# Reordering the start of a delta-rule attention and two mixture-of-experts layers on one Trainium2 core

## The chip, the cores and the metric

The kernel runs on one core of one Trainium2 chip. The metric is the device time of one launch in microseconds (us). TensorE is called PE here, its weight load PEld, VectorE DVE, ScalarE ACT, GpSimd POOL and SyncE SP. SPq and ACTq are the issue slots of SP and ACT, in which those engines start DMA transfers.

## The reference, cut to what matters

Three layers follow one another. The first is a linear attention with a delta rule, over 4 batches x 8 heads, 768 positions, head size 48. The second sends its output through 8 experts, all of them for all tokens, weighted by a matrix that is balanced 8 times over rows and columns. The third sends every token through its best expert only.

```python
def _attn_ref(q, k, v, beta):
    k_n = k / (np.linalg.norm(k, axis=-1, keepdims=True) + 1e-06)
    for t in range(S):
        y[:, :, t] = einsum('bhd,bhde->bhe', q[:, :, t], state)
        v_old = einsum('bhde,bhd->bhe', state, kt)
        state = state + bt * einsum('bhd,bhe->bhde', kt, vt - v_old)

def _moe_ref(x, w_gate, w1, w2):            # N, D, E, F = 3072, 384, 8, 1024
    P = np.exp(logits - logits.max())
    for _ in range(8):
        P /= P.sum(1); P /= P.sum(0); P *= N / E
    for e in range(E):
        out += P[:, e:e + 1] * (np.maximum(x @ w1[e], 0.0) @ w2[e])

def _moe2_ref(x, expert_emb, tau, w1, w2):
    # cosine score against 8 embeddings, argmax, softmax weight of the winner
    out[mask] = gate_w[mask, None] * (np.maximum(x[mask] @ w1[e], 0.0) @ w2[e])
```

## The kernel before, in words

The attention is cut into NC = 12 chunks of C = 64 positions; the 32 heads lie as 16 pairs, two heads on the 128 partitions. For a chunk `c` the kernel makes:

- `gram(c)`, the 64x64 products of keys with keys (64 small matmuls into `psA`), which `scale(c, ...)` on DVE multiplies by `gam` and stores as `an`; SP writes it to memory in `store_a(c)`.
- `mix(c)`, the products of keys with queries (64 small matmuls into `psH` or `psB`). ACT copies the result to `mt[c]` in `copy_m(c)`, DVE masks it in `mask(c)`.
- The inverse of a triangular matrix. Two chunks together are a group `n`. SP loads their 32x32 blocks in `load_blocks(n)` (tile `sa`, 8 loads of 64 KB), DVE solves in `solve(n, first, end)` (31 steps of two instructions, lines 945 and 948), ACT transposes in `transpose_blocks(n)` (tile `sr`), SP stores in `store_inverse(n)`, and `load_inverse(engine, c)` loads the blocks back in another layout (tiles `rs`, `ts`, 6 loads of 64 KB a chunk).
- `cross(c)` and `corner(c)`, which make the off-diagonal block of the inverse, then `write_values(c)`, `outputs(c)`, `keys_state(c)`, which carry the state from chunk to chunk, and `transpose_y(c)`, `scores(c)` with `high_x` on ACT and `low_x` on DVE, which hand the chunk's output to the second layer.

`gam` holds the inverse squared norms of the keys times beta. The keys come in PARTS = 6 parts of 768 KB (`load_parts(m)`, tiles `kq`); ACT squares them (`squares_of(m)`), DVE sums them (`reduce_part(m)`), ACT takes the root (`root(i)`), DVE finishes (`norms(i)`). Parts 3 to 5 are finished together, in `norms(3)`.

The first expert of the second layer is computed chunk by chunk beside the attention: `block_hidden(k)` (nine matmuls, line 1392) and `block_give(k)` (six matmuls, line 1407), 8 of each for a chunk. Each weight is used as a high and a low part: `split_first(half, layer)` on ACT makes the high part from the loaded `fh` (line 641), the one on DVE the low part (line 980). The other seven experts and the third layer follow.

The order is written out by hand. Before the main loop each engine runs a prologue; then every engine walks `for s in range(LAST)` and does at step `s` what the tables `AT_KS`, `AT_X`, `AT_O`, `AT_W`, `AT_Y`, `AT_T`, `AT_SC`, `AT_GRAM`, `AT_MIX`, `AT_MASK`, `AT_PART`, `AT_SPLIT` and `SOLVE` place there. Each engine is in order, and engines meet only through semaphores. Chunk 0 has `cross` at s=0, `corner` at 1, `write_values` at 2, `outputs` at 3; chunk 1 has `cross` at 2, `corner` at 3, `keys_state` at 4, `outputs` at 6; `block_hidden(0)` is at s=6. `gram(4)`, `gram(5)` and `gram(6)` are at 8, 9 and 14. `mix(4)` to `mix(7)` are at 1, 2, 4 and 5. Within one step of PE the block products come first, then `keys_state`, `transpose_y`, `scores`, `cross`, `corner`, `write_values`, `outputs`, `gram`, `mix`.

Keys and queries for `gram` and `mix` of the first eight chunks come in pairs of chunks, 1 MB each, into the buffers `kP[0..2]` and `qP[0..1]`: pair 2 of the queries reuses `qP[0]`, pair 3 reuses `kP[1]` and `qP[1]`. From `gram(6)` on, keys come chunk by chunk into `kTs`.

SP issues nearly all transfers in one order. In the main loop it has at s=9 `store_inverse(1)`, at s=10 `store_a(4)`, then these lines, then `load_inverse` for chunks 2 and 3, at s=11 `store_a(5)`, and at s=12 `load_blocks(2)` and the load of `kTs` that `gram(6)` waits for:

```python
if s == AT_GRAM[5] + 1:
    sp.wait_ge(g_done, 6)
    sp.wait_ge(m_done, 8)
    sp.wait_ge(y_done, 2)
    for m in range(3, PARTS):
        load_parts(m)
```

Of the kernel before, what the change touches and what calls it, by code (L numbers as in the profile page):

```python
# [15 lines left out]
P = 128  # L16
C = 64
NC = S // C
# [4 lines left out]
KC = DM // P  # L23
# [44 lines left out]
AT_SOLVED = [None, 8] + [16 * n - 9 for n in range(2, NG)]  # L68
AT_MASK = [None, 2] + [t + 1 for t in AT_KS[2:]]

EARLY = 4
AT_MIX = [None] * EARLY + [1, 2, 4, 5] + [AT_KS[c - 4] + 4 for c in range(8, NC)]
AT_GRAM = [None] * EARLY + [8, 9, AT_KS[2] + 3] + [AT_KS[c - 4] + 2 for c in range(7, NC)]
AT_PART = [None] * 3 + [11, 12, 13]
AT_SPLIT = {2: (0, 0), 3: (0, 1), 5: (1, 0), 6: (1, 1)}
AT_SPLIT_END = 7
# [36 lines left out]
def build(nc, kT, qT, kn, vn, beta, consts, wg, w1, w2, emb, tau, v1, v2, out):  # L113
# [5 lines left out]
    with ExitStack() as ctx:  # L119
# [6 lines left out]
        def keep(name, shape, dt=F32, at=None):  # L126
            if at is None:
                at = top[0]
                top[0] += -(-4 * int(np.prod(shape[1:])) // 32) * 32
            return nc.alloc_sbuf_tensor_at(name, shape, dt, offset=at)  # L130
# [4 lines left out]
        for i in range(2):  # L135
# [13 lines left out]

        part, pair = 4 * 2 * NJ * D, 4 * GR * NJ * C  # L150
        kq = [keep(f"kq{i}", [P, 2 * NJ, D], at=at) for i, at in
              enumerate([w_at, w_at + part, w_at + 3 * part] + [x_at + (2 + i) * part for i in range(3)])]
        assert part == 4 * 2 * KC * SLOT
# [8 lines left out]
        kP = [keep(f"kP{i}", [P, GR, NJ, C], at=x_at + i * pair) for i in range(KP)]  # L162
        qP = [keep(f"qP{i}", [P, GR, NJ, C], at=x_at + NC * (chunk_x - chunk_m) + 8 * chunk_m + i * pair) for i in range(2)]

# [154 lines left out]
        def mix_bank(c):  # L319

            return psA if c >= 8 else psB if c in (1, 3) else psH
# [45 lines left out]
        with nc.Block() as block:  # L367
            @block.sync
            def _(sp):
# [7 lines left out]
                def store_a(c):  # L377
                    sp.wait_ge(an_ready, c + 1)
                    sp.dma_start(a_dram[c], an[a_buffer(c)][:, :, :]).then_inc(an_out[a_buffer(c)], 16)
# [49 lines left out]
                load_pair(qP[1], qT, 1, s_qP[1])  # L429
                load_first(0)  # L430
                for c in range(2):
                    load_corner(c)
                store_a(2)
                sp.dma_start(kns[:, :, :], kn[0]).then_inc(s_kn, 16)
                sp.dma_start(kTs[:, :, :], kT[1]).then_inc(s_kT, 16)
                sp.dma_start(qTs[:, :, :], qT[1]).then_inc(s_qT, 16)
                load_parts(2)
                sp.dma_start(embs[0:E, :], emb).then_inc(emb_in, 16)
                sp.dma_start(wgs[:, :, :], wg.rearrange("(k p) e -> p k e", p=P)).then_inc(s_wg, 16)
                sp.dma_start(taus[:, :], tau.to_broadcast([P, 1])).then_inc(tau_in, 16)  # L440
                load_pair(kP[2], kT, 2, s_kP[2])
                sp.wait_ge(m_done, 2)
                load_pair(qP[0], qT, 2, s_qP[0])
                store_inverse(0)
                store_a(3)
                load_blocks(1)
                load_first(1)
                sp.wait_ge(vs_ready, 1)
# [3 lines left out]
                load_pair(kP[1], kT, 3, s_kP[1])  # L452
                load_pair(qP[1], qT, 3, s_qP[1])
                for s in range(LAST):
                    if s - 2 in AT_GRAM[EARLY:6]:
                        store_a(AT_GRAM.index(s - 2))
                    if s - 2 in AT_GRAM[6:NC]:
                        store_a(AT_GRAM.index(s - 2))
                    if s == AT_GRAM[5] + 1:
                        sp.wait_ge(g_done, 6)  # L460
                        sp.wait_ge(m_done, 8)
                        sp.wait_ge(y_done, 2)
                        for m in range(3, PARTS):
                            load_parts(m)
                    if s == 12:
# [139 lines left out]
            def _(act):  # L605
# [17 lines left out]
                def copy_m(c):  # L623
                    act.wait_ge(m_done, c + 1)
                    act.activation(mt[c][:, :, :], mix_bank(c)[:, :, :], ACT.Copy).then_inc(mt_copied, 1)

# [22 lines left out]
                root(1)  # L649
                for c in range(1, EARLY):  # L650
                    copy_m(c)
                squares_of(2)
                transpose_blocks(0)
                for c in range(2):
                    load_inverse(act, c)

# [205 lines left out]
            def _(dve):  # L862
# [169 lines left out]
                solve(0, 0, BS - 1)  # L1032
                scale(3, psA)

                first_iteration = AT_SC[-1] + 2
                for s in range(LAST):
# [8 lines left out]
                    if k is not None:  # L1045
                        low(k)
                    if s == AT_SPLIT_END - 2:
                        reduce_part(2)
                    if s == AT_SPLIT_END + 1:
# [222 lines left out]
            def _(pe):  # L1272
# [149 lines left out]
                pe.wait_ge(mt_copied, 2)  # L1422
                mix(3)
                pe.wait_ge(s_const, 16)
                pe.wait_ge(s_wg, 16)
                for s in range(LAST):
# [28 lines left out]
                    if s in AT_MIX:  # L1455
                        c = AT_MIX.index(s)
                        if c >= 8:
                            pe.wait_ge(an_ready, c + 1)
                        else:
                            pe.wait_ge(mt_copied, c - 1 if c == 4 else c)  # L1460
                        mix(c)
# [192 lines left out]
```

## Time and profile before

| what | value |
| --- | --- |
| time, median of 3 runs | 2381.35 us (2379.86 to 2382.3) |
| the profiled execution's own time | 2386.1 us |
| its span, first to last instruction | 2384.2 us |
| PE busy in the span | 2253.3 us (95%) |
| DVE, ACT, POOL busy in the span | 1020.9, 612.3, 106.2 us |
| mean granted clock of PE, share of full speed | 0.959 |

A start is counted from the span's start. "Idle before" is the time in which the engine did nothing ahead of an instruction, with what ended it. The granted clock of PE has two levels, 2.4 GHz (1.00 in a row) and 1.2 GHz (0.50); a value between them is a mean over a stretch. Times of a page belong to one execution, the median to unprofiled ones.

### The profile page before, as it was taken

The numbers are of one execution on the slowest core, as the hardware profiler recorded it, in microseconds if no ns is written. First come the engines' busy times: TensorE is split into PE (matmuls) and PEld (weight loads), VectorE is DVE, ScalarE is ACT, GpSimd is POOL, SyncE is SP. The second block draws the span as 40 slices with busy tenths as digits, with TensorE's granted clock in tenths as the row PEclk, the third lists the DMA queues.
The fourth block names the chain that finished last, engine by engine and source line by source line (L and its number), as shares of the span: only waits on it lengthen the run. The fifth ranks groups of instructions, "written<-read, shape, count | busy, mean of one in ns | idle before, by whom it ended". The sixth has DMA issues, their size and how long they took to land.

```text
span 2384.2 us, 43062 instructions
## 1 busy us (share of the span) xinstructions
PE 2253.3 (95%) x18100; PEld 2090.3 (88%) x18100; DVE 1020.9 (43%) x1831; ACT 612.3 (26%) x1021; POOL 106.2 (4%) x106
## 2 busy tenths in 40 slices
PE   3779999999999999999999999999999996899998
PEld 3768898998999998999899899989999886899998
DVE  6655555435333332333333232332323225566664
ACT  2322222322111111111111111111111112566664
POOL 0000000000000000000000000000000000222221
PEclk7779999999999999999999999999999997899999
DMA  8544434331000000000000000000000012666651
GB/s 283 128 140 130 128 115 116 110 143 53 1 27 1 27 10 18 27 1 27 1 27 27 1 27 1 27 27 1 1 1 1 23 31 96 218 217 219 232 194 61
DMA packets 153379, 173.93 MB, mean 73 GB/s; under 512 B 82124, under 2 KB 113008, under 8 KB 153218
## 3 DMA queue, kind: packets, MB, share of 16 engines
q1 hardware_dynamic: 142018, 158.50, 20.7%
q0 software_dynamic: 4864, 12.20, 1.4%
q8 instruction: 137, 2.24, 0.4%
q10 hardware_dynamic: 6336, 0.79, 0.3%
q14 instruction: 24, 0.20, 0.0%
HBM read 145.50 MB, written 28.71 MB: 73 GB/s over the span
## 4 chain that ended last, share of the span: by engine, by line
PE 89%; DVE 5%; DMA 2%; SPq 1%; issue 1%; ACT 0%; ACTq 0%; POOL 0%; POOLq 0%; DVEq 0%
PE psA L1491 21%; PE psH L1506 15%; PE psB L1491 8%; PE psB L1506 7%; PE psY L1506 7%; PE psY L1600 7%; PE psH L1392 4%; PE psA L1276 4%; PE psA L1587 3%; PE psY L1407 3%; PE psB L1587 3%; PE psB L1365 1%; PE psB L1375 1%; DVE products L945 1%; DVE sx L948 1%
## 5 line engine op out<-in xcount | busy, mean ns | idle before, releaser
L1491 PE MATMUL psA<-X,wh 128*128 128x512 f32 x1440 | 456.3, 398 | 6.2 <-DVE wl L1092 4.1
L1099 DVE SCALAR_TENSOR_TENSOR hl<-psA,hh 128x512 fp32r<-128x512 f32 x240 | 166.1, 692 | 649.5 <-ACT hh L769 649.4
L769 ACT ACTIVATE hh<-psA 128x512 fp32r<-128x512 f32 x240 | 143.8, 599 | 856.6 <-PE psA L1491 856.6
L1491 PEld LDWEIGHTS psA<-X,wh 128*128 128x128 f32 x1440 | 270.6, 191 | 53.3 <-issue 7.7
L1491 PE MATMUL psA<-X,wl 128*128 128x512 f32 x720 | 289.2, 402 | 0.0
L1506 PE MATMUL psH<-wh,hh 128*128 128x384 f32 x672 | 228.4, 340 | 0.0
L1506 PE MATMUL psH<-wh,hl 128*128 128x384 f32 x672 | 227.2, 338 | 0.0
L1506 PE MATMUL psH<-wl,hh 128*128 128x384 f32 x672 | 225.8, 336 | 0.0
L1099 DVE SCALAR_TENSOR_TENSOR hl<-psB,hh 128x512 fp32r<-128x512 f32 x96 | 66.5, 693 | 277.2 <-ACT hh L769 277.2
L1491 PE MATMUL psB<-X,wh 128*128 128x512 f32 x576 | 179.2, 392 | 0.0
L1223 DVE TENSOR_TENSOR vl<-vs,vh 128x768 fp32r<-128x768 f32 x152 | 145.1, 957 | 57.4 <-ACT vh L806 55.8
L1491 PEld LDWEIGHTS psA<-X,wl 128*128 128x128 f32 x720 | 137.5, 191 | 29.8
L769 ACT ACTIVATE hh<-psB 128x512 fp32r<-128x512 f32 x96 | 57.5, 599 | 344.0 <-PE psB L1491 344.0
L806 ACT ACTIVATE vh<-vs 128x768 fp32r<-128x768 f32 x152 | 127.3, 840 | 15.0 <-DMA vs<-v_d 14.9
L1506 PEld LDWEIGHTS psH<-wh,hh 128*128 128x128 f32 x672 | 126.3, 188 | 0.0
L1506 PEld LDWEIGHTS psH<-wl,hh 128*128 128x128 f32 x672 | 126.1, 188 | 0.0
L1506 PEld LDWEIGHTS psH<-wh,hl 128*128 128x128 f32 x672 | 125.9, 187 | 0.0
L1491 PEld LDWEIGHTS psB<-X,wh 128*128 128x128 f32 x576 | 106.7, 188 | 17.7
L1392 PE MATMUL psH<-X,wh 128*128 128x256 f32 x576 | 116.3, 298 | 1.2 <-DVE X L975 1.2
L1491 PE MATMUL psB<-X,wl 128*128 128x512 f32 x288 | 114.0, 396 | 0.0
L1506 PE MATMUL psB<-wh,hl 128*128 128x384 f32 x336 | 113.9, 339 | 0.0
L1506 PE MATMUL psB<-wl,hh 128*128 128x384 f32 x336 | 113.7, 338 | 0.0
(235 smaller groups left out, 4247.8 us busy)
## 6 DMA issues: line engine op xcount, KB each, us to landing
vs<-v_d SPq DMA_DIRECT2D x38, 768.0 KB, 6.2
vs<-v_d SPq DMA_DIRECT2D x19, 1536.0 KB, 12.2
ws<-w_d SPq DMA_DIRECT2D x28, 768.0 KB, 6.2
kT<-kT_d SPq DMA_DIRECT2D x17, 512.0 KB, 4.3
qT<-qT_d SPq DMA_DIRECT2D x15, 512.0 KB, 5.1
a_scratch<-an SPq DMA_DIRECT2D x12, 512.0 KB, 3.5
kq<-kn_d SPq DMA_DIRECT2D x6, 768.0 KB, 8.1
vn<-vn_d SPq DMA_DIRECT2D x12, 384.0 KB, 4.4
```

The source lines that it names most:

```text
L769: act.activation(hh[kk % 3][:, :], ps_h[kk % (2 if last else 3)], ACT.Relu).then_inc(hh_ready, 1)
L806: act.activation(piece(to, q), piece(src, q), ACT.Copy).then_inc(vh_ready, 1)
L945: dve.tensor_tensor(pv, sa[n % 2][:, s + 1:BS, s:s + 1].to_broadcast([P, rows, cols]), sx[:, s:s + 1, 0:cols].to_broadcast([P, rows, cols] ...
L1099: dve.scalar_tensor_tensor(hl[b][:, :], ps_h[bank], 0.0, hh[b][:, :].bitcast(F32), ALU.max, ALU.subtract).then_inc(hl_ready, 1)
L1223: dve.tensor_tensor(piece(to, q), piece(src, q), piece(high, q).bitcast(F32), ALU.subtract).then_inc(vl_ready, 1)
L1276: mm = pe.matmul(ps[g * C:g * C + M, j, at:at + W], lhsT[g * C:g * C + K, j, 0:M], rhs[g * C:g * C + K, j, 0:W], start=True, stop=True, sk ...
L1392: mm = pe.matmul(ps_b[k % 2], a[half][:, c, col], X[:, u, b, c, :], start=(n == 0), stop=(n == 3 * KC - 1))
L1407: mm = pe.matmul(ps_u[i], a[k % 4][:, i * P:(i + 1) * P], b[half][:, f % FB, :], start=(f == 0 and n == 0), stop=(f == KF - 1 and n == 2))
L1491: mm = pe.matmul(to, a[half][:, c, col], X[:, 2 * g:2 * g + 2, b, c, :], start=(n == 0), stop=(n == 3 * KC - 1))
L1506: mm = pe.matmul(ps_y[i][:, 0:DM], a[kk % 3][:, q], b[half][:, f, :], start=(f == 0 and n == 0), stop=(f == FB - 1 and n == 2))
L1587: mm = pe.matmul(ps_g[f % 4], a[par][:, c, f * P:(f + 1) * P], b[par][:, c, :], start=(n == 0), stop=(n == 3 * KC - 1))
L1600: mm = pe.matmul(ps_o[s], a[f % 4][:, q], b[par][:, f, :], start=(f == 0 and n == 0), stop=(f == KF - 1 and n == 2))
```

## The change

In PE's prologue `mix(4)` and `mix(5)` are added behind `mix(3)`, ahead of `cross(0)`; `mix(6)` and `mix(7)` take their places at s=1 and 2. For that SP loads pair 2 right behind query pair 1, and ACT copies all six results in its prologue. ACT and DVE split the first half of the first expert's weights in their prologues, and DVE masks chunk 1 and reduces part 2 there; the second half is split at s=8 and 9. SP now issues the six inverse loads of chunk 1 that ACT issued, ahead of `load_blocks(1)`; the loads of `qTs` for chunk 1 and of the second half of the weights (`load_first(1)`) move behind pair 3. Parts 3 to 5 of the keys are loaded at s=7 instead of 10, into other addresses, and worked on at s=9 to 11 instead of 11 to 13, so that `norms(3)` is at s=13 instead of 15. `copy_m(8)` has a wait for all six reductions.

```diff
--- before.py
+++ after.py
@@ -66,13 +66,13 @@
 SOLVE_SECOND = [4, 4, 4, 4, 3, 3, 3, 3, 3]
 SOLVE_THIRD = [2, 3, 3, 3, 3, 3, 3, 3, 3, 3, 2]
 AT_SOLVED = [None, 8] + [16 * n - 9 for n in range(2, NG)]
-AT_MASK = [None, 2] + [t + 1 for t in AT_KS[2:]]
+AT_MASK = [None, None] + [t + 1 for t in AT_KS[2:]]
 
 EARLY = 4
-AT_MIX = [None] * EARLY + [1, 2, 4, 5] + [AT_KS[c - 4] + 4 for c in range(8, NC)]
+AT_MIX = [None] * 6 + [1, 2] + [AT_KS[c - 4] + 4 for c in range(8, NC)]
 AT_GRAM = [None] * EARLY + [8, 9, AT_KS[2] + 3] + [AT_KS[c - 4] + 2 for c in range(7, NC)]
-AT_PART = [None] * 3 + [11, 12, 13]
-AT_SPLIT = {2: (0, 0), 3: (0, 1), 5: (1, 0), 6: (1, 1)}
+AT_PART = [None] * 3 + [9, 10, 11]
+AT_SPLIT = {8: (1, 0), 9: (1, 1)}
 AT_SPLIT_END = 7
 AT_EMB = 18
 SPILLED = 10
@@ -148,8 +148,9 @@
         end_dense = top[0]
 
         part, pair = 4 * 2 * NJ * D, 4 * GR * NJ * C
+        late_at = x_at + NC * (4 * 2 * KC * SLOT - 4 * NJ * C) + 8 * 4 * NJ * C
         kq = [keep(f"kq{i}", [P, 2 * NJ, D], at=at) for i, at in
-              enumerate([w_at, w_at + part, w_at + 3 * part] + [x_at + (2 + i) * part for i in range(3)])]
+              enumerate([w_at, w_at + part, w_at + 3 * part, late_at, late_at + part, x_at + 4 * part])]
         assert part == 4 * 2 * KC * SLOT
         fh1 = [keep(f"fh1_{i}", [P, KC, FH], at=wl_at + 4 * KC * FH * i) for i in range(2)]
         fh2 = [keep(f"fh2_{i}", [P, FB, DM], at=wl_at + 8 * KC * FH + 4 * FB * DM * i) for i in range(2)]
@@ -160,7 +161,7 @@
         chunk_x, chunk_m = 4 * 2 * KC * SLOT, 4 * NJ * C
         mt = [keep(f"mt{c}", [P, NJ, C], at=x_at + NC * (chunk_x - chunk_m) + c * chunk_m) for c in range(NC)]
         kP = [keep(f"kP{i}", [P, GR, NJ, C], at=x_at + i * pair) for i in range(KP)]
-        qP = [keep(f"qP{i}", [P, GR, NJ, C], at=x_at + NC * (chunk_x - chunk_m) + 8 * chunk_m + i * pair) for i in range(2)]
+        qP = [keep(f"qP{i}", [P, GR, NJ, C], at=late_at + i * pair) for i in range(2)]
 
         top[0] = base
         kTs, qTs = keep("kT", [P, NJ, C]), keep("qT", [P, NJ, C])
@@ -427,41 +428,42 @@
                 load_blocks(0)
                 sp.dma_start(vns[:, :, :], vn[0]).then_inc(s_vn, 16)
                 load_pair(qP[1], qT, 1, s_qP[1])
-                load_first(0)
+                load_pair(kP[2], kT, 2, s_kP[2])
+                sp.wait_ge(m_done, 2)
+                load_pair(qP[0], qT, 2, s_qP[0])
                 for c in range(2):
                     load_corner(c)
                 store_a(2)
+                load_first(0)
+                load_parts(2)
                 sp.dma_start(kns[:, :, :], kn[0]).then_inc(s_kn, 16)
                 sp.dma_start(kTs[:, :, :], kT[1]).then_inc(s_kT, 16)
-                sp.dma_start(qTs[:, :, :], qT[1]).then_inc(s_qT, 16)
-                load_parts(2)
                 sp.dma_start(embs[0:E, :], emb).then_inc(emb_in, 16)
                 sp.dma_start(wgs[:, :, :], wg.rearrange("(k p) e -> p k e", p=P)).then_inc(s_wg, 16)
                 sp.dma_start(taus[:, :], tau.to_broadcast([P, 1])).then_inc(tau_in, 16)
-                load_pair(kP[2], kT, 2, s_kP[2])
-                sp.wait_ge(m_done, 2)
-                load_pair(qP[0], qT, 2, s_qP[0])
                 store_inverse(0)
                 store_a(3)
+                load_inverse(sp, 1)
                 load_blocks(1)
-                load_first(1)
                 sp.wait_ge(vs_ready, 1)
                 sp.dma_start(vns[:, :, :], vn[1]).then_inc(s_vn, 16)
                 sp.wait_ge(m_done, 4)
                 sp.wait_ge(g_done, 4)
                 load_pair(kP[1], kT, 3, s_kP[1])
                 load_pair(qP[1], qT, 3, s_qP[1])
+                sp.dma_start(qTs[:, :, :], qT[1]).then_inc(s_qT, 16)
+                load_first(1)
                 for s in range(LAST):
                     if s - 2 in AT_GRAM[EARLY:6]:
                         store_a(AT_GRAM.index(s - 2))
                     if s - 2 in AT_GRAM[6:NC]:
                         store_a(AT_GRAM.index(s - 2))
-                    if s == AT_GRAM[5] + 1:
-                        sp.wait_ge(g_done, 6)
+                    if s == 7:
                         sp.wait_ge(m_done, 8)
+                        load_parts(3)
+                        load_parts(4)
                         sp.wait_ge(y_done, 2)
-                        for m in range(3, PARTS):
-                            load_parts(m)
+                        load_parts(5)
                     if s == 12:
                         load_blocks(2)
                     if s in range(24, 16 * NG - 24, 16):
@@ -622,6 +624,8 @@
 
                 def copy_m(c):
                     act.wait_ge(m_done, c + 1)
+                    if c == 8:
+                        act.wait_ge(s_red, PARTS)
                     act.activation(mt[c][:, :, :], mix_bank(c)[:, :, :], ACT.Copy).then_inc(mt_copied, 1)
 
                 def transpose_blocks(n):
@@ -647,12 +651,13 @@
                 squares_of(1)
                 copy_m(0)
                 root(1)
-                for c in range(1, EARLY):
+                for c in range(1, 6):
                     copy_m(c)
+                split_first(0, 0)
+                split_first(0, 1)
                 squares_of(2)
                 transpose_blocks(0)
-                for c in range(2):
-                    load_inverse(act, c)
+                load_inverse(act, 0)
 
                 def high_x(c):
                     act.wait_ge(t_done, c + 1)
@@ -1031,6 +1036,10 @@
                 mask(0)
                 solve(0, 0, BS - 1)
                 scale(3, psA)
+                mask(1)
+                split_first(0, 0)
+                split_first(0, 1)
+                reduce_part(2)
 
                 first_iteration = AT_SC[-1] + 2
                 for s in range(LAST):
@@ -1044,8 +1053,6 @@
                     k = block_of(s)
                     if k is not None:
                         low(k)
-                    if s == AT_SPLIT_END - 2:
-                        reduce_part(2)
                     if s == AT_SPLIT_END + 1:
                         norms(2)
                     if s - 1 in AT_PART:
@@ -1421,6 +1428,10 @@
                 mix(2)
                 pe.wait_ge(mt_copied, 2)
                 mix(3)
+                pe.wait_ge(mt_copied, 3)
+                mix(4)
+                pe.wait_ge(mt_copied, 5)
+                mix(5)
                 pe.wait_ge(s_const, 16)
                 pe.wait_ge(s_wg, 16)
                 for s in range(LAST):
@@ -1457,7 +1468,7 @@
                         if c >= 8:
                             pe.wait_ge(an_ready, c + 1)
                         else:
-                            pe.wait_ge(mt_copied, c - 1 if c == 4 else c)
+                            pe.wait_ge(mt_copied, c)
                         mix(c)
                     if s == AT_SC[-1]:
                         pe.wait_ge(rt, RT_EN)
```

## Rows read from the trace of the kernel before

**Rows 1.** Busy time of each engine by stretch; last columns: PE clock, DMA share, GB/s

```profile
36.60:65.10 28.50, 0.01 (x1) 0.04 (x3) 15.23 (x40) 4.46 (x3) 0.00 (x0) 0.55 1.00 249
...
68.00:72.00 4.00, 0.47 (x18) 0.48 (x20) 3.79 (x9) 1.18 (x2) 0.89 (x1) 0.50 1.08 375
...
125.00:154.50 29.50, 20.47 (x331) 19.34 (x332) 11.89 (x18) 9.19 (x13) 0.00 (x0) 0.79 0.78 220
600.00:2384.00 1784.00, 1741.06 (x9464) 1605.97 (x9463) 695.36 (x1098) 448.08 (x761) 80.49 (x78) 0.98 0.16 52
```

**Rows 2.** Timeline of PE, 60 to 170 us: start, duration, instruction, idle before

```profile
65.09 1.92 PE L1334 MATMUL psB<-rs,ao 32*32 32x32 f32 x64 [28.50 <-issue]
...
79.28 1.92 PE L1334 MATMUL psB<-rs,ao 32*32 32x32 f32 x64 [2.23 <-DMA rs<-r_scratch]
...
106.43 0.48 PE L1392 MATMUL psH<-X,wh 128*128 128x256 f32 x2 [1.17 <-DVE X L975]
...
118.25 2.08 PE L1276 MATMUL psA<-kP 48*64 48x64 f32 x64
...
125.05 3.68 PE L1276 MATMUL psA<-kP 48*64 48x64 f32 x64 [2.42 <-DVE an L927]
...
154.52 3.68 PE L1276 MATMUL psA<-kT 48*64 48x64 f32 x64 [7.28 <-DMA kT<-kT_d]
...
168.39 0.66 PE L1407 MATMUL psY<-wh,hhA 128*128 128x384 f32 x1 [4.96 <-DVE y0s L967]
```

**Rows 3.** Timeline of DVE, 60 to 166 us

```profile
65.33 0.21 DVE L945 TENSOR_TENSOR products<-sa,sx 128x31 f32<-128x31 f32 x1 [8.34 <-issue]
...
101.66 1.75 DVE L980 TENSOR_TENSOR wl<-fh,wh 128x1536 fp32r<-128x1536 f32 x1
103.33 2.23 DVE L975 TENSOR_TENSOR X<-xf,X 128x768 fp32r<-128x768 f32 x1
105.48 1.74 DVE L889 TENSOR_REDUCE n<-kq 128x32 f32<-128x1536 f32 x1
...
118.65 0.95 DVE L975 TENSOR_TENSOR X<-xf,X 128x768 fp32r<-128x768 f32 x1
...
161.21 0.20 DVE L898 TENSOR_SCALAR n<-n 128x96 f32<-128x96 f32 x1
...
164.43 1.22 DVE L927 TENSOR_TENSOR an<-psA,gam 128x1024 f32<-128x1024 f32 x1
```

**Rows 4.** Timeline of SP's DMA issues, 60 to 230 us: start, time of issuing

```profile
63.09 0.47 SPq L375 DMA_DIRECT2D qP<-qT_d  x1
...
125.55 0.33 SPq L403 DMA_DIRECT2D r_scratch<-sr  x1
...
128.77 2.16 SPq L372 DMA_DIRECT2D kq<-kn_d  x3
...
142.88 1.03 SPq L361 DMA_DIRECT2D rs<-r_scratch  x2
...
150.15 0.48 SPq L474 DMA_DIRECT2D kT<-kT_d  x1
...
220.57 0.32 SPq L361 DMA_DIRECT2D rs<-r_scratch  x1
...
227.68 1.02 SPq L361 DMA_DIRECT2D rs<-r_scratch  x2
```

**Rows 5.** Timeline of ACT with its DMA issues, 50 to 71 us

```profile
50.97 1.95 ACT L634 ACTIVATE sr<-sx 128x1024 f32<-128x1024 f32 x1 [5.46 <-DVE sx L948]
...
63.17 7.05 ACTq L361 DMA_DIRECT2D rs<-r_scratch  x2
```

**Rows 6.** The query pairs' tile, 0 to 160 us: time from issue to landing

```profile
DMA to landing us min/median/max: 6.9/9.8/14.9
```

**Rows 7.** The chain that ended last, 52 to 56 us

```profile
52.95 2.68 DMA r_scratch<-sr
```

**Rows 8.** Timeline of POOL, 0 to 210 us

```profile
102.70 2.05 POOL L561 TENSOR_TENSOR vn<-vn,br 128x768 f32<-128x768 f32 x1 [29.83 <-DMA vn<-vn_d]
```

## The prediction

> **What bounds the kernel now.** I read the stretches first. From 600 us on PE is busy in 1741.1 of 1784 us [rows 1], and the change touches nothing there; that part can only shift as a block. Then I looked on PE's timeline for idle time in the first 170 us, where all moved work lies. PE has nothing to do from 36.6 to 65.1 us, while DVE solves the first group (15.2 us busy) and ACT is busy for 4.5 us [rows 1]. The other gaps are a wait for the inverse of chunk 1 at 79.28 us (2.23 us), for DVE's `low_x` at 106.43 (1.17), for DVE's `scale(4)` at 125.05 (2.42), for the keys of `gram(6)` at 154.52 (7.28) and for DVE's `unit_out(0)` at 168.39 (4.96) [rows 2]. So the start is bound by a chain that changes engine at every step, and what counts is which wait ends last at each of these places. Behind 168 us PE, the engine that ends last, keeps its order and its work, so I carry the shift at 168.39 to the end of the span unchanged.
>
> **Part 1, the products ahead of `cross(0)`, and pair 3.** `mix(4)` and `mix(5)` fall into the idle 28.5 us of PE: 3.68 us each at the slower clock (a `gram` has the same 64 matmuls and lasts that long in [rows 2]), so they cost nothing. ACT gets two copies, two splits and nothing else new before its transpose at 50.97 us. It is free 5.46 us ahead of that now [rows 5] and idle for most of the 30 us before (4.5 us busy of 28.5 [rows 1]), which covers it if the weights land in time; with the cover gone each us late would be a us on everything behind. DVE's moved mask (the size of the 1.22 us at 164.43), two splits and one reduction (1.2 + 2 x 1.75 + 1.74 = 6.5 us) fit ahead of 65.33 us, up to which it is idle for 8.34 us behind its memsets [rows 3].
>
> At s=1 PE now meets `mix(6)`, which stands in front of `cross(1)` and needs pair 3. This is the new wait, and I look for what ends it. Before, the query pair 3 was issued at 63.09 us [rows 4] and landed 14.9 us later (the longest of the four [rows 6]), at 78.0. Ahead of it in SP's queue stood 1.5 MB of weights, `load_first(1)`, now behind it. At 375 GB/s [rows 1] they take 4.2 us. The small loads ahead of the pair are 20 in either order (12 of inverses, 8 of blocks). So pair 3 lands at 73.8, `mix(6)` runs to 77.5, and `cross(1)` starts 1.8 us earlier than at 79.28; its own inverse loads, now ahead of the pair in the queue, are there by then. The bounds: not before `corner(0)` is done, about 70 us (65.09 and 1.92 for `cross(0)` [rows 2], ACT's copy, as much again for `corner(0)`; ACT no longer issues loads until 70.22 [rows 5]), and not behind the 78.0 of before if only the order changes. I take 73.8, since both ends need the same bytes to move. Behind the waiting `mix(6)` stand all of PE's work, and through it everything. The blocks of group 1 land some 4 us later than for 65.33 us, as six more loads are ahead of them; DVE's first 16 steps then end before 85, when PE has delivered nothing to it yet. The cost is nothing.
>
> **Part 2, s=4 to s=9.** PE loses two products of 2.08 us here [rows 2]. DVE loses more: the split at 101.66 (1.75 us), the reduction at 105.48 (1.74) and both splits of the second half (2 x 1.75), which now stand behind `scale(4)` and `scale(5)` [rows 3]. Without the split, `low_x(0)` starts at 101.66 instead of 103.33. There it took 2.23 us, the next one 0.95 [rows 3], and POOL worked from 102.70 on [rows 8]; if it starts at 101.66 it is done before POOL begins. So `block_hidden(0)` starts at 102.7 instead of 106.43, 3.7 us earlier; if the stall of 1.28 us stays on it, 2.4. I take 3.7, the sum so far being 5.5. The first split stood where DVE waited for PE, and its removal is counted at nothing.
>
> The Trainium skill, in "SBUF — State Buffer", section "SBUF: two separate sides", calls the port pair of VectorE and GpSimd an exclusive lock held for the whole instruction. The 2.23 against 0.95 us agree with it; whoever starts first wins, which is the order assumed here, and with POOL first the sum would be 1.3 us less.
>
> From `block_hidden(0)` to the end of `gram(4)` (106.43 to 120.33) PE ran without a wait and does so again, 5.5 us earlier. `scale(4)` was then late by DVE's backlog: PE waited 2.42 us. With 5.2 us less on DVE it waits only for what hangs on the last block: its copy, `low(3)` and `scale(4)`, the last alone 1.22 us (as at 164.43 [rows 3]), less what PE does beside it. What stays of the 2.42 lies between nothing and all; I take 1.0, near the 1.22. So `gram(5)` starts at 118.1, 6.9 us earlier. The two splits now run on DVE beside `gram(5)` and the blocks behind it, and the first is needed at `block_hidden(4)`, 2.1 to 3.7 us after `scale(4)` has ended, against 1.75 for its run. That costs nothing; uncovered it would cost up to 1.75.
>
> **Part 3, SP's queue up to `gram(6)`.** `gram(6)` waits for a load issued at 150.15 [rows 4]. SP came to it late. The end of the solve and the transposed blocks come about 7.0 us earlier by part 2 (125.55 becomes 118.5). Their store lands 2.68 us after its issue [rows 7], at 128.2 before, but SP then issued the three parts of the keys until 130.93 and only then the twelve inverse loads: 2.7 us go away. These twelve took from 130.93 to 143.91, 13.0 us, with 2.3 MB of keys in front of them; the next time, without, 8.1 us (220.57 to 228.70) [rows 4]. I take 8.1, saving 4.9; the other bound is 0, if the issue is slow by itself. Then `store_a(5)`, `load_blocks(2)` and the keys follow unchanged. Sum: 7.0 + 2.7 + 4.9 = 14.6 us, `gram(6)` at 139.9. Is PE there? Its work from 125.05 to 154.5 is 20.5 us [rows 1]; from 118.1 that ends at 138.6. So the load still ends last, by a little over a us, and a slip of PE beyond that would be the next bound. The parts' own loads now go out at s=7, where SP has little else to issue; one of them stands ahead of `kns` and `qTs` of chunk 2, which nobody reads before `outputs(2)` at s=18. The added wait of `copy_m(8)` is at s=31, long after the reductions.
>
> On DVE the reductions of parts 3 to 5 now stand at s=10 to 12. The first (1.74 us) is ahead of `scale(5)`, which SP's `store_a(5)` needs only when its twelve loads are out, so it is hidden.
>
> **Part 4, `unit_out(0)`.** Between `gram(6)` and 168.39 lay `norms(3)`, from 161.21 to 164.43 [rows 3], 3.2 us in the middle of the chain to `unit_out(0)`, for which PE waited 4.96 us. At s=13 it now runs while PE waits for the keys. The gain is 3.2, bounded by 0 if the reduction or root comes late. Sum: 14.6 + 3.2 = 17.8 us. The profiled span would go from 2384.2 to 2366.4 us, its own time from 2386.1 to 2368.3. The median was 4.75 below that own time, so I subtract from the median: 2381.35 - 17.8 = 2363.55, say 2363.6 us.
>
> **The rivals.**
> A: the twelve loads are slow by themselves. For it: the last two of ACT's twelve took 7.05 us [rows 5]; against: the 8.1 us of the second set. It takes back 4.9: 2368.5 us.
> B: pair 3 lands where it did, at 78.0, because the small loads and not the bytes set it. It takes back 4.2, and everything behind it shifts: 2367.8 us.
> C: PE's clock stays up. `gram(6)` took 3.68 us behind an idle 7.28, the same product 2.08 at 118.25 behind busy work [rows 2]. The wait shrinks to about 1.3 us. At full clock `gram(6)` gains 1.6 us, and the block products behind it and at 168 us some 2.4 more (an estimate, by the same ratio from about 5.5 us of slow work): 4.0 in all, 2359.6. Against it, `gram(5)` was slow behind only 2.42 us of idle.
> D, the other side: `mix(6)` is a new gate. Every us that pair 3 is late beyond 73.8 is a us lost; at 91.6 the gain is gone, from 96.4 on the kernel is slower by over 0.2%. SP has 14 small loads ahead of the pair, from 55.63 on, when the first inverse has landed [rows 7]. At the pace of ACT's last two, 3.5 us each [rows 5], they end at 104.7, and with 6.7 us for the 2.5 MB behind them `mix(6)` starts at 111.4: 19.8 us slower, 2401.2. At 0.5 us each, as the last two of [rows 4], they end near 63.
> E: nothing is won: the earlier start is given back to waits at s=19 and later: 2381.4.
>
> On C the Trainium skill ("TensorE: Matmul & The Clock Gate", section "What's actually happening") says that the slow clock is the default and activity releases it. By that, shorter waits help beyond their length, and C would be the outcome at 2359.6; the trace agrees in that long gaps are followed by slow products.
>
> **How the numbers follow.** Forecast 0.56, A 0.12, B 0.10, C 0.12, D 0.04, E 0.06. All but D and E are faster by over 0.2% (4.8 us, about what a measurement of this kernel can tell from no change): faster 0.90, same 0.06, slower 0.04. The low end is C with an early pair 3 (2 us more), 2357.5; the high end is A and B together, 2372.7. It leaves out D and E.
>
> **What would show it.** In the new trace: `mix(4)` and `mix(5)` before 50 us; `mix(6)` starting near 74 behind a wait for the query or key pair; no wait for inverse loads at `cross(1)`; `block_hidden(0)` near 101; `gram(5)` near 118; twelve loads in about 8 us; `gram(6)` near 140 still behind a wait for keys; the first product into `psY` of chunk 1 near 150.6 with under 2 us of idle. It would be wrong if the transpose at 50.97 moved, if `mix(6)` started behind 78, or if a gap opened behind 170 us that is not there now.

## The result and the profile after

The changed kernel took 2364.76 us (median of 4 runs, 2361.99 to 2368.86) against 2381.82 us before: ratio 0.9931, 95% interval 0.9914 to 0.9948, 17.1 us less. Run again unaltered it gave 2363.22 us against 2381.26, ratio 0.9927 (0.9914 to 0.9941), 18.0 us less. The forecast was 2363.6 us, 17.8 less.

The timeline of PE after, 0 to 175 us, has these rows where [rows 2] had theirs; `mix(4)` and `mix(5)` come first, `cross(0)` third, `mix(6)` fourth, and the last is `cross(3)`, which stood at 197.17 us before:

```profile
36.29 2.10 PE L1283 MATMUL psH<-qP,kP 48*64 48x64 f32 x64
39.51 2.08 PE L1283 MATMUL psH<-qP,kP 48*64 48x64 f32 x64 [1.12 <-ACT mt L629]
60.53 1.92 PE L1341 MATMUL psB<-rs,ao 32*32 32x32 f32 x64 [18.95 <-issue]
...
71.64 3.68 PE L1283 MATMUL psH<-qP,kP 48*64 48x64 f32 x64 [5.98 <-DMA qP<-qT_d]
75.24 1.92 PE L1341 MATMUL psB<-rs,ao 32*32 32x32 f32 x64
...
95.27 1.50 PE L1327 MATMUL psB<-wgs,xf 128*128 128x8 f32 x12 [0.90 <-ACT xf L671]
...
99.38 0.79 PE L1399 MATMUL psH<-X,wh 128*128 128x256 f32 x2
...
117.56 2.08 PE L1283 MATMUL psA<-kP 48*64 48x64 f32 x64 [1.12 <-DVE an L932]
...
137.63 2.76 PE L1283 MATMUL psA<-kT 48*64 48x64 f32 x64 [1.71 <-DMA kT<-kT_d]
...
147.23 0.41 PE L1414 MATMUL psY<-wh,hhA 128*128 128x384 f32 x1 [2.64 <-DVE y0s L972]
...
174.20 1.92 PE L1341 MATMUL psB<-rs,ao 32*32 32x32 f32 x64 [3.23 <-DVE pm L1071]
```

Each gap of [rows 2] is shorter or gone. New are 5.98 us for pair 3 ahead of `mix(6)`, 0.90 us ahead of `scores(0)`, 0.80 us ahead of `keys_state(2)` at 124.86, and the 1.12 us ahead of `mix(5)`, which costs nothing, as PE waits 18.95 us behind it. The last row waits for the same 3.23 us as in the kernel before, so from there the order runs as it did.

SP's issues after, 117 to 134 us, against [rows 4]: the blocks are stored 7.8 us earlier, no keys stand behind them, and the twelve inverse loads run from 120.91 to 127.07, in 6.2 us:

```profile
117.73 0.33 SPq L404 DMA_DIRECT2D r_scratch<-sr  x1
...
120.91 0.32 SPq L362 DMA_DIRECT2D rs<-r_scratch  x1
...
126.05 1.02 SPq L362 DMA_DIRECT2D rs<-r_scratch  x2
...
133.37 0.48 SPq L476 DMA_DIRECT2D kT<-kT_d  x1
```

DVE after around `low_x(0)` (line 980 of the changed kernel), against [rows 3]; and POOL's product of the same time, against [rows 8]:

```profile
98.09 0.95 DVE L980 TENSOR_TENSOR X<-xf,X 128x768 fp32r<-128x768 f32 x1
...
99.92 1.56 DVE L950 TENSOR_TENSOR products<-sa,sx 128x231 f32<-128x231 f32 x1
```

```profile
99.54 1.68 POOL L563 TENSOR_TENSOR vn<-vn,br 128x768 f32<-128x768 f32 x1 [33.09 <-DMA vn<-vn_d]
```

`low_x(0)` ran before POOL began and took 0.95 us; the stall went to a product of the solve (1.56 us, its neighbours 0.40). The Trainium skill ("SBUF — State Buffer", section "SBUF: two separate sides") says that whichever of the two engines starts first gets the shared port pair for its whole instruction. The trace agrees: the product that began 0.38 us behind POOL's start took 1.16 us longer than its neighbours.

### The profile page after: what moved, and what is told of

The parts are those of the page before. It is cut to its first block, busy times and chain, and to the rows that moved or that the text cites. A ratio compares the mean times of both kernels' runs of the same rounds, so it can differ in the third digit from the quotient of the medians.

```text
span 2360.2 us, 43063 instructions
## 1 busy us (share of the span) xinstructions
PE 2249.2 (95%) x18100; PEld 2086.9 (88%) x18100; DVE 1021.7 (43%) x1831; ACT 611.9 (26%) x1021; POOL 105.2 (4%) x106
## 4 chain that ended last, share of the span: by engine, by line
PE 90%; DVE 5%; DMA 2%; SPq 1%; issue 1%; ACT 1%; POOL 0%; POOLq 0%; DVEq 0%; ACTq 0%
PE psA L1502 21%; PE psH L1517 15%; PE psB L1502 8%; PE psB L1517 7%; PE psY L1517 7%; PE psY L1611 7%; PE psH L1399 4%; PE psA L1598 4%; PE psB L1598 3%; PE psY L1414 3%; PE psA L1283 3%; PE psB L1372 1%; PE psB L1382 1%; SPq L398 1%; DVE products L950 1%
## 5 line engine op out<-in xcount | busy, mean ns | idle before, releaser
L811 ACT ACTIVATE vh<-vs 128x768 fp32r<-128x768 f32 x152 | 127.1, 839 | 15.1 <-DMA vs<-v_d 15.0
## 6 DMA issues: line engine op xcount, KB each, us to landing
vs<-v_d SPq DMA_DIRECT2D x19, 1536.0 KB, 12.1
```

The source lines that it names most:

```text
L811: act.activation(piece(to, q), piece(src, q), ACT.Copy).then_inc(vh_ready, 1)
```

## How far two executions differ

The first profiled execution of the kernel before took 2386.1 us, 5 us above its median, and that of the changed kernel 2361.99, 3 us below. A shift read from the two alone comes out at 24 us. So both kernels were run and profiled once more.

> The kernel before, unaltered, once more, for a second profile. Its first profiled execution took 2386.1 us, its median is 2381. If the 5 us lie in the start, cross(3) starts at 190 to 193 us here instead of 197.2, and its span ends near 2379.

> The changed kernel once more, unaltered, for a second profile and a tighter ratio. If the 23 us by which cross(3) (line 1341 after the third chunk) was earlier in the first profile (174.2 against 197.2 us) belongs to the change, it starts at 173 to 176 us again and the ratio is near 0.990. If 5 to 6 us of it were the luck of two single executions, as the medians (17 us apart) say, it starts at 176 to 180 us in this profile, or the later part of the span is longer, and the ratio is 0.9925 to 0.9935.

The second execution of the kernel before took 2379.18 us, with a span of 2377.3; `cross(3)` started at 193.92 us instead of 197.17, so 3 of the 7 us between the two lie in the first 197 us; the start lies 0.9 us above the expected range. The second of the changed kernel had a span of 2359.9 and `cross(3)` at 175.80, as expected if all of the shift belonged to the change, while its ratio, 0.9927, is that of the other case. Both profiled executions of the changed kernel (2361.99 and 2361.72 us) were faster than their medians. Start times in us, as means of two executions each:

| place | before | after | earlier by | forecast |
| --- | --- | --- | --- | --- |
| `cross(1)` | 79.28, 77.73 | 75.24, 76.43 | 2.7 | 1.8 |
| `block_hidden(0)` | 106.43, 103.99 | 99.38, 100.56 | 5.2 | 5.5 |
| `gram(5)` | 125.05, 122.96 | 117.56, 117.93 | 6.3 | 6.9 |
| `gram(6)` | 154.52, 151.49 | 137.63, 138.19 | 15.1 | 14.6 |
| first product of `block_give(8)` | 168.39, 165.36 | 147.23, 148.83 | 18.8 | 17.8 |
| `cross(3)` | 197.17, 193.92 | 174.20, 175.80 | 20.5 | 17.8 |
| end of the span | 2384.2, 2377.3 | 2360.2, 2359.9 | 20.7 | 17.8 |

Single executions differ by 1 to 4 us at these places, so a row confirms a term only to about that. The timed runs say 17.1 and 18.0 for the whole.

## Experiments

All were timed against the kernel before on the same chip; all but the second profile of the kernel before have an interval. These intervals reach some 3 us to either side, so a difference between two changed kernels, taken from their ratios, is known to 4 or 5 us only. Where it is no larger, the start times in the profiles have to carry the reading.

**Parts of the keys alone.** In the kernel before:

```diff
-AT_PART = [None] * 3 + [11, 12, 13]
+AT_PART = [None] * 3 + [9, 10, 11]
-                    if s == AT_GRAM[5] + 1:
-                        sp.wait_ge(g_done, 6)
+                    if s == 7:
...
```

with the new addresses and the wait in `copy_m(8)`.

> The kernel before with parts 3 to 5 of the keys alone moved (their new addresses, loads at s=7, squares at s=9 to 11, norms(3) at s=13). Theory (SP's queue): gram(6) loses its late keys, 7.6 us of queue time, but cannot start before PE is ready, 7.3 us earlier than 154.5; norms(3) leaves the chain to unit_out(0), 3.2 us. Sum 10.5, less up to 1.7 for the reduction ahead of scale(5): 2371 to 2373 us. Rival (the queue is not the gate, the gain comes from the products and the splits): at most 3 us, 2379 us.

Measured: 2373.75 us, ratio 0.9970 (0.9958 to 0.9982), 7.1 us faster. `gram(6)` started at 146.59 us behind a wait of 0.92, and `block_give(8)` waited 2.98 us instead of 4.96 or 5.19. The mechanism holds; the time is 0.8 us above the expected range, and the wait at `block_give(8)` shrank by 2.0 to 2.2 us where 3.2 were expected.

**The parts put back** into the changed kernel (the reverse of that diff, the addresses kept).

> The changed kernel with parts 3 to 5 loaded at s=10 and worked on at s=11 to 13 again. Theory (SP's queue): the twelve inverse loads take 13 us again instead of 8, and 2 to 3 us go to issuing the keys; gram(6) starts 7 to 8 us later than in the changed kernel, and norms(3) adds 3.2: 2374 to 2376 us. Rival (other waits end last there, the parts are hidden): within 3 us of the changed kernel.

Measured: 2376.72 us, ratio 0.9977 (0.9968 to 0.9986), 12 us slower than the changed kernel by the ratios, where 10 to 11 were expected; so the rest of the change alone is worth 5.5 us (3.3 to 7.6 by the interval). SP's issues of this kernel, 121 to 146 us:

```profile
121.89 0.33 SPq L404 DMA_DIRECT2D r_scratch<-sr  x1
...
123.84 1.63 SPq L373 DMA_DIRECT2D kq<-kn_d  x3
125.59 0.40 SPq L362 DMA_DIRECT2D rs<-r_scratch  x1
...
126.64 4.17 SPq L362 DMA_DIRECT2D rs<-r_scratch  x1
...
131.52 4.31 SPq L362 DMA_DIRECT2D rs<-r_scratch  x3
...
137.46 1.02 SPq L362 DMA_DIRECT2D rs<-r_scratch  x2
...
143.76 1.79 SPq L476 DMA_DIRECT2D kT<-kT_d  x1
```

Single loads take up to 4.17 us to issue here, and the twelve end at 138.48, 12.9 us after they began; with the parts at s=7 they took 6.2. `gram(6)` waited 5.91 us for its keys and started at 149.13, 27.4 us behind `gram(5)` where it was 20.1 and 20.3; that is the expected 7 to 8 us. This excludes rival A, that the loads are slow by themselves. The two halves alone give 7.1 and 5.5 us, together 17 to 18. With the parts alone PE itself came late to `gram(6)` (146.59, wait 0.92); with the rest alone its keys did (149.13, wait 5.91); only with both does it start at 137.63 and 138.19.

**The late `norms(3)`.**

```diff
-AT_PART = [None] * 3 + [9, 10, 11]
+AT_PART = [None] * 3 + [11, 12, 13]
```

> The changed kernel with the early loads of parts 3 to 5, but squares, reductions and norms(3) at s=11 to 15 as before. Theory: gram(6) stays (137 to 139 us), the 3.2 us of norms(3) come back between gram(6) and unit_out(0), PE's wait for y0s grows by as much: 3.2 us slower than the changed kernel. Rival: the wait for y0s has another cause (the 3 solve steps and the low part), then no difference.

Measured: 2370.41 us, ratio 0.9952 (0.9938 to 0.9965), about 6 us slower than the changed kernel. The wait for `y0s` is 5.87 us instead of 2.64 and 2.20, 3.2 to 3.7 more, as expected. The rest is not explained in full. In this profile `gram(5)` was late already (121.37 us), behind a longer fall of PE's clock, of which below. But `gram(6)`, expected at 137 to 139, came at 143.69 behind a wait of 4.80 us for its keys, 22.3 us behind `gram(5)` instead of 20.1 and 20.3; whether the edit has a part in that is open.

**The weights ahead of pair 3 again.**

```diff
                 load_blocks(1)
+                load_first(1)
...
-                load_first(1)
                 for s in range(LAST):
```

> The changed kernel with the load of the second half of the first expert's weights (1.5 MB) ahead of pair 3 again. Theory (bytes ahead of the pair, each us of mix(6) is a us of the kernel): mix(6) starts 4.2 us later, and so does everything behind, the end too: 4 us slower than the changed kernel. Rival (the small loads set the landing, or the lateness is taken up by a later wait): mix(6) or at least gram(6) where it was, no difference.

Measured: 2370.25 us, ratio 0.9949 (0.9935 to 0.9964), 5.2 us slower than the changed kernel. `mix(6)` started at 78.30 us instead of 71.64 and 72.82, behind a wait of 11.19 us, and `gram(6)` at 144.94 instead of 137.63 and 138.19, 6.8 to 7.3 later. So `mix(6)` is a gate that passes its lateness on, and 1.5 MB ahead of the pair cost 5.5 to 6.7 us there, more than the 4.2 of the forecast.

**Chunk 1's inverse loads on ACT again.**

```diff
-                load_inverse(sp, 1)
...
-                load_inverse(act, 0)
+                for c in range(2):
+                    load_inverse(act, c)
```

> The changed kernel with the six inverse loads of chunk 1 on ACT's queue again. Theory: ACT issues until 60 to 66 us, behind big transfers up to 70, so the copy between cross(0) and corner(0) is late, but mix(6) waits for pair 3 anyway (71.6 us): no difference or, as SP gets to pair 3 some 3 us sooner, 1 to 3 us faster. Rival (the move is what made cross(1) free of its wait): cross(1) waits for inverse loads again, 2 us or more slower.

Measured: 2368.89 us, ratio 0.9949 (0.9937 to 0.9961), 5.2 us slower; the theory of the expectation was wrong, and its rival came out. PE's timeline of this kernel, 60 to 83 us:

```profile
65.31 1.92 PE L1341 MATMUL psB<-rs,ao 32*32 32x32 f32 x64 [23.17 <-issue]
70.98 1.92 PE L1349 MATMUL psB<-xx,ts 32*32 32x32 f32 x64 [3.76 <-ACT xx L728]
72.83 3.68 PE L1283 MATMUL psH<-qP,kP 48*64 48x64 f32 x64
80.97 1.91 PE L1341 MATMUL psB<-rs,ao 32*32 32x32 f32 x64 [4.46 <-DMA rs<-r_scratch]
```

Pair 3 is there when `mix(6)` comes, but `cross(1)` waits 4.46 us for its inverse loads, and starts 4.5 to 5.7 us later than in the changed kernel. The move from ACT to SP is what frees it. On SP's queue these loads stand ahead of the big transfers; on ACT's they run beside them, and I take their late landing to come from that, though only the landing was seen. The same move frees chunk 0: `cross(0)` follows the store of its inverse by 12.3 us here (12.1 and 12.2 in the kernel before) and by 9.2 and 9.1 in the changed kernel, and `corner(0)` waits 3.76 us for ACT's copy here instead of 1.29.

**`mix(6)` and `mix(7)` behind `cross(1)`.**

```diff
-AT_MIX = [None] * 6 + [1, 2] + ...
+AT_MIX = [None] * 6 + [2, 3] + ...
```

> The changed kernel with mix(6) and mix(7) one step later (s=2 and 3), so that cross(1) and write_values(0) no longer stand behind the wait for pair 3. Theory (mix(6) is the new gate): cross(1) starts near 66 to 68 us instead of 75.2, the wait moves behind write_values(0) and shrinks; what comes after is 4 to 5 us earlier, the kernel 4 us faster than the changed one. Rival (the gate is something else, a load of cross(1) or DVE's solve): under 1 us.

Measured: 2359.78 us, ratio 0.9908 (0.9893 to 0.9922), about 4.5 us faster than the changed kernel, where 4 were expected; the intervals of the two just overlap. `cross(1)` started at 68.67 us, a little above the expected 66 to 68, and `mix(6)` at 73.97 without a wait.

**The second splits ahead of `scale(4)` again.**

```diff
-AT_SPLIT = {8: (1, 0), 9: (1, 1)}
+AT_SPLIT = {5: (1, 0), 6: (1, 1)}
```

> The changed kernel with the two splits of the second half of the weights at s=5 and 6 again, ahead of scale(4). Theory (DVE's backlog): 3.5 us more on DVE before scale(4); PE's wait ahead of gram(5) grows from 1.1 us by 2 to 3.5, and all behind it is that much later, the kernel 2 to 3.5 us slower. Rival (the queue of SP alone sets gram(6)): gram(5) late, gram(6) in place, under 1 us.

Measured: 2367.24 us, ratio 0.9939 (0.9924 to 0.9954), 2.8 us slower by the middle of the interval, which overlaps that of the changed kernel. PE waited 2.41 us ahead of `gram(5)` (at 120.75) instead of 1.12; from the start of `gram(4)` to that of `gram(5)` it took 6.80 us instead of 5.51. The mechanism is seen at 1.3 us of the 2 to 3.5; on the end the runs don't settle it. `gram(6)` was not in place but at 142.65, so the rival, that SP's queue alone sets it, did not come out.

**PE's clock where two products are gone.** Here are the busy times by stretch, with the clock granted to PE in the third column from the right: 97 to 103 and 103 to 114 us of the kernel before, of the changed one, and of the one with the parts put back, in this order.

```profile
97.00:103.00 6.00, 6.00 (x146) 5.69 (x143) 5.62 (x9) 2.68 (x3) 0.30 (x1) 1.00 0.46 156
103.00:114.00 11.00, 9.83 (x287) 9.54 (x284) 10.66 (x19) 5.78 (x6) 1.74 (x1) 1.00 0.16 53
```

```profile
97.00:103.00 6.00, 6.00 (x123) 5.78 (x121) 5.76 (x12) 1.20 (x2) 1.68 (x1) 0.72 0.86 322
103.00:114.00 11.00, 11.00 (x254) 10.91 (x248) 8.03 (x25) 4.61 (x7) 0.00 (x0) 1.00 0.45 158
```

```profile
97.00:103.00 6.00, 6.00 (x82) 5.89 (x81) 5.73 (x12) 1.04 (x2) 1.66 (x1) 0.61 0.26 88
103.00:114.00 11.00, 11.00 (x219) 10.72 (x219) 5.41 (x15) 2.59 (x5) 0.00 (x0) 0.75 0.25 85
```

The clock fell to 0.50 (1.2 GHz) for 3.4 us in the changed kernel and for 10.2 in the other, behind the 0.90 us wait and the twelve products of `scores(0)`, where `mix(6)` had stood ahead of `scores(0)` and `mix(7)` behind it. It fell there in all seven profiles with both products at s=1 and 2, in four of them for 3.4 us, in two for 10.2 and in one for 13.7, and in none of the three in which they stand at the old places. From the start of `keys_state(1)` to that of `gram(4)` it took 20.5 us in the changed kernel, 23.5 with the parts put back and 25.1 with the loads on ACT, without any difference in PE's work.

Three more kernels put `mix(7)` at s=4, between `transpose_y(0)` and `scores(0)`, where the wait is; `mix(6)` stands at s=3, 2 and 1 in them, so that the third moves `mix(7)` alone:

```diff
+AT_MIX = [None] * 6 + [3, 4] + ...
+AT_MIX = [None] * 6 + [2, 4] + ...
+AT_MIX = [None] * 6 + [1, 4] + ...
```

> The changed kernel with mix(6) at s=3 and mix(7) at s=4, between transpose_y(0) and scores(0), where PE waits 0.9 us for ACT's copy. Theory: as with mix(6) and mix(7) at s=2 and 3, cross(1) starts near 68.5 us, and one product fills the wait ahead of scores(0): equal to that variant or up to 1 us faster, 2358 to 2360 us. Rival: chunk 1 waits longer for the copies, up to 2 us slower than that variant.

> The changed kernel with mix(6) at s=2, behind write_values(0), and mix(7) at s=4, between transpose_y(0) and scores(0). Theory: 2358 to 2360 us, as above, block_hidden(0) near 93 us. Rival: copy and product at s=4 delay scores(0) and chunk 1's values by more than the wait they fill, 1 to 2 us slower.

> The changed kernel with mix(7) alone moved, from s=2 to s=4. In every profile of the changed kernel PE's granted clock fell to 0.50 near 97 us for 3 to 13 us, where mix(6) and mix(7) stood before, and in none of the kernel before. Theory: sparse work of PE there lets the clock fall; with mix(7) put back there is no fall from 96 to 110 us, or a shorter one, and the runs scatter less (3 us instead of 7). In sum 1 to 3 us faster than the changed kernel, and gram(4) at most 22.5 us behind the start of keys_state(1) (20.5 in the shortest case). Rival: the fall is a chance of the execution; the clock falls here as well and the time is that of the changed kernel or up to 2 us more.

| kernel | median, us | ratio (interval) | `cross(1)` | `block_give(8)` | clock, 97 to 103 us |
| --- | --- | --- | --- | --- | --- |
| changed, again | 2363.22 | 0.9927 (0.9914 to 0.9941) | 76.43 | 148.83 | 0.72 |
| `mix` 6, 7 at s=2, 3 | 2359.78 | 0.9908 (0.9893 to 0.9922) | 68.67 | 141.01 | 1.00 |
| at 3, 4 | 2360.78 | 0.9901 (0.9882 to 0.9919) | 68.51 | 141.58 | 1.00 |
| at 2, 4 | 2357.79 | 0.9889 (0.9872 to 0.9905) | 68.66 | 141.79 | 1.00 |
| at 1, 4 | 2361.87 | 0.9900 (0.9882 to 0.9918) | 77.22 | 146.16 | 1.00 |

(The last three ran on a chip where the kernel before took 2384.13 us; the ratios are what to compare.) The kernels with `mix(6)` at s=2 or 3 run 5 to 8 us earlier here, so that 97 to 103 us is other work in them; but their clock stays at 1.00 from 84 to 129 us without a break. These are the stretches of the kernel with `mix(7)` alone moved, to s=4:

```profile
97.00:103.00 6.00, 5.79 (x174) 5.47 (x171) 5.66 (x15) 1.20 (x2) 1.49 (x1) 1.00 0.55 222
103.00:114.00 11.00, 11.00 (x182) 10.86 (x179) 7.80 (x27) 5.20 (x9) 0.00 (x0) 1.00 0.45 158
```

The fall is gone there and in the other three. But the kernel with `mix(6)` and `mix(7)` at s=2 and 3 has no product in that wait, just as the changed kernel. These are its rows for `mix(7)`, `keys_state(1)`, `transpose_y(0)` and `scores(0)`, and its stretch around them:

```profile
84.61 2.04 PE L1283 MATMUL psH<-qP,kP 48*64 48x64 f32 x64
86.50 2.02 PE L1283 MATMUL psA<-st,kT 48*64 48x48 f32 x64
88.49 0.87 PE L1320 MATMUL psB<-cst,ysb 128*128 128x128 f32 x6
90.26 1.50 PE L1327 MATMUL psB<-wgs,xf 128*128 128x8 f32 x12 [0.90 <-ACT xf L671]
```

```profile
82.00:97.00 15.00, 13.82 (x349) 13.21 (x346) 9.05 (x16) 4.58 (x6) 1.73 (x1) 0.95 0.58 191
```

The wait, its length and the work from `keys_state(1)` on are those of the changed kernel, yet the clock rose to 1.00 at 83.5 us and did not fall. So the thin stretch alone does not make the fall. What the profiles show is that the place of `mix(7)` matters: with it at s=2 the clock fell in seven profiles of seven, at s=3, 4 or 5 in none of seven, though only one of these is of the kernel that moves nothing else. Where it fell it had risen 0.3 to 1.7 us ahead of `keys_state(1)`, in this kernel 3.0 us, with `mix(7)` in between; whether that is the reason is open.

This kernel also shows what a short fall costs. From `keys_state(1)` to `gram(4)` it took 20.0 us with the same work and no fall, against 20.5 and 20.6 in the two profiles of the changed kernel; with `mix(7)` in the wait it took 20.55. A long fall costs 3.5 to 5 us. In the median nothing of this is clear: 0.9900 and 0.9927 have overlapping intervals. The expected smaller scatter did not come: the four runs of the kernel with `mix(7)` alone moved, which has no fall in its profile, lie 7.4 us apart, those of the changed kernel 6.9 in its first measurement and 3.0 in its second.

With `mix(6)` and `mix(7)` at 3 and 4 the time was 0.8 us above the expected range, with 2 and 4 it was 0.2 below; `block_hidden(0)` came at 92.19 there, where 93 was expected. This last one has an interval wholly below that of the changed kernel and the lowest ratio of all: 1.1% faster than before, 0.4% faster than the change.

## Why the prediction was right

- **Pair 3** was forecast at 73.8 us and came at 71.64 and 72.82. Rival B (78.0) fell. That `mix(6)` is a new gate whose lateness passes through, the base of rival D, is shown by the weights put ahead of it; in its place it costs about 4.5 us against the order with `mix(6)` behind `write_values(0)`. The lateness of D itself did not come: the 14 small loads were issued by 61.4 us, near the 63 that the prediction gave as the other case (its 104.7 for the slow case is 104.6 by its own terms). The term for `cross(1)`, 1.8 us, came out at 2.7. Its cause was more than the order of the bytes: without the move of the inverse loads `cross(1)` would have waited 4.5 us in any case. The prediction said only that these loads would be there by then. It also did not count what the move gives chunk 0: `cross(0)` came at 60.53 and 61.75 instead of 65.09 and 63.67, and `corner(0)` at 63.74 and 64.95 instead of 71.53 and 70.23. The wait for pair 3 hides that, and only the kernels with `mix(6)` further back use it (`cross(1)` at 68.5 to 68.7).
- **DVE's backlog.** 3.7 us at `block_hidden(0)` became 2.6 in the means. The step named the right wait, and `low_x(0)` did run ahead of POOL, but the fall of the clock slowed PE's work at 97 us: `write_values(1)` took 2.75 and 3.6 us there instead of 2.07, on average the 1.1 us that are missing. The prediction did not see that its new places for the products would let the clock fall. What the removed split, the removed reduction and the two removed products gave each was not run apart. For `gram(5)` the wait was taken as 1.0 and was 1.12.
- **SP's queue.** 7.0 + 2.7 + 4.9 was the sum of the step. In the means of the two pairs of profiles the store came 6.6 us earlier (7.8 and 5.4), the way from it to the first inverse load became 1.7 shorter (2.3 and 1.1), and the twelve loads took 6.2 us instead of 13.0, 6.8 less; the 8.1 assumed for them was 1.9 too much. PE was the next bound by 1.7 to 2.0 us, forecast as a little over one. In the means `gram(6)` moved by 15.1, forecast 14.6: one term was too small and two were too large. That the sum is so close is in part luck.
- **`norms(3)`.** 3.2 forecast, 3.7 in the means (18.8 less 15.1). The wait itself shrank by 2.3 and 3.0 us (4.96 and 5.19 to 2.64 and 2.20), and did not get under 2 us as forecast; the rest is PE's work between `gram(6)` and `block_give(8)`, which ran faster. Putting `norms(3)` back lengthened the wait by 3.2 to 3.7.
- **C**, the clock staying up, came in part. `gram(6)` took 2.76 and 3.68 us, and the first product of `block_give(8)` 0.41 instead of 0.66; but a new fall at 97 us stood against it. Losing 3 to 14 us of full clock there is the case that the prediction lacked. That the fall's length makes the scatter of the runs is not shown, and the kernel with `mix(7)` alone moved, which has no fall in its profile and scatters as widely, speaks against it.
- **Behind 168 us** the shift was to stay. In the timed runs it did (17.1 and 18.0 against 17.8), and rival E fell; the 20.7 of the spans rests on two executions of each kernel. From `block_give(8)` to `cross(3)` PE has the same order in all kernels, and took 28.8 and 28.6 us before, 27.0 in both profiles of the changed kernel, and between 27.0 and 31.2 in the others, so the 1.7 us won there say nothing of the change.

## What to carry to other kernels

Where a start-up chain changes engine at every step, list the waits and ask of each edit which wait ends last once it is made: two halves of this change were worth 7.1 and 5.5 us alone and 17 to 18 together. A product moved ahead should not stand in front of work that is ready sooner than its data; one step later was worth about 4 us more. And moving TensorE's work can cost its clock further on, where no wait has grown: read the granted clock after the edit beside the waits. Here, with one product one or two steps later, it stayed up.

## What the runs showed of the hardware

- The time that a small load takes to issue depends on what was issued before it. Twelve loads of 64 KB took 6.2 us behind three stores of 0.5 MB, and 12.9 with 2.3 MB of loads issued just before as well, single ones up to 4.17 us. The Trainium skill ("DMA: Bandwidth & Descriptors", section "Issuing engines are not separate DMA queues") calls the sequencer time that a second issuing engine saves usually small beside the transfer itself. Here the place in the queue mattered: the same six loads issued by SP ahead of the big transfers instead of by ACT beside them brought `cross(1)` 4.5 to 5.7 us forward, and the kernel 5.2 us by the ratios.
- PE's granted clock fell from 1.00 to 0.50 behind a wait of only 0.90 us and the twelve small products after it, in seven profiles of seven. In the kernel with `mix(6)` and `mix(7)` at s=2 and 3, with the same wait and the same work from `keys_state(1)` on, it stayed at 1.00 in the one profile taken.
- The fall lasted 3.4 us in four of these profiles, 10.2 in two and 13.7 in one, with the same work of PE there.
